# Attention in units of 64 tokens of all four batches, in place of 256 tokens of one, in a fused attention and two-MLP kernel

## The reference

```python
f = 1.0 / (1.0 + np.exp(-f_logit))
for t in range(S):                      # gated linear attention
    state = f[:, :, t, :, None] * state + np.einsum('bhd,bhe->bhde', k[:, :, t], v[:, :, t])
    y[:, :, t] = np.einsum('bhd,bhde->bhe', q[:, :, t], state)
x = y.transpose(0, 2, 1, 3).reshape(3072, 384)
x = ((1/(1+np.exp(-(x @ w_gate)))) * (x @ w_val)) @ w_out      # 384 -> 1536 -> 384
h = x @ w_in                                                   # 384 -> 2048
out = (h * (1/(1+np.exp(-1.702 * h)))) @ w_out2                # 2048 -> 384
```

## Time and profile before

| | us |
|---|---|
| three runs, median | 945.4 (943.34 to 945.67) |
| the profiled execution | 943.24 |
| its span | 941.5 |
| TensorE busy in the span | 928.0 (99%), 7197 matmuls |
| VectorE, ScalarE, GpSimd busy | 453.3, 375.1, 114.3 |
| first matmul of the first MLP | at 27.71 |

### The profile page before, as it was taken

One profiled execution on the slowest core, in us unless ns is written; L12 is line 12 of the kernel. 1 busy time (PEld: TensorE's weight loads), 2 busy tenths in 40 slices (PEclk: granted clock), 3 DMA queues, 4 the chain that ended last, 5 costly groups with the idle time before them and its releaser, 6 DMA issues.

```text
span 941.5 us, 18155 instructions
## 1 busy us (share of the span) xinstructions
PE 928.0 (99%) x7197; PEld 776.5 (82%) x7197; DVE 453.3 (48%) x886; ACT 375.1 (40%) x917; POOL 114.3 (12%) x125
## 2 busy tenths in 40 slices
PE   7999999999999999999999999999999999999997
PEld 5899988888888888888888888888888888888886
DVE  7787775456546544753333243343443443343433
ACT  4765654444444434443334342333232233332332
POOL 4222221101112110210014420000000000000000
PEclk8999999999999999999999999999999999999999
DMA  5852322112211221120123320020100200200000
GB/s 144 244 158 71 89 68 74 43 47 82 56 46 41 76 59 44 56 55 12 59 84 102 101 67 1 1 68 1 45 23 1 68 1 1 67 1 1 35 1 36
DMA packets 44008, 52.36 MB, mean 56 GB/s; under 512 B 8464, under 2 KB 33808, under 8 KB 43920
## 3 DMA queue, kind: packets, MB, share of 16 engines
q1 hardware_dynamic: 41488, 43.53, 16.2%
q10 hardware_dynamic: 2432, 7.62, 2.7%
HBM read 36.96 MB, written 9.44 MB: 49 GB/s over the span
## 4 chain that ended last, share of the span: by engine, by line
PE 94%; DVE 2%; SPq 1%; DMA 1%; issue 1%; ACT 0%; DVEq 0%; ACTq 0%
PE up_ps L1094 17%; PE up_ps L1096 17%; PE up_ps L1095 17%; PE out_ps L1094 13%; PE out_ps L1095 12%; PE out_ps L1096 12%; PE att_ps L1042 2%; PE att_ps L1064 1%; PE att_ps L1054 1%; PE att_ps L1087 1%; PE turn_ps L1021 1%; DMA x_raw<-y_t 1%; PE out_ps L1006 1%; SPq L411 0%; PE att_ps L1076 0%
## 5 line engine op out<-in xcount | busy, mean ns | idle before, releaser
L1094 PE MATMUL up_ps<-x_hi,w_hi 128*128 128x512 f32 (+1 forms) x792 | 293.3, 370 | 0.1
L1096 PE MATMUL up_ps<-x_hi,w_lo 128*128 128x512 f32 (+1 forms) x792 | 293.0, 370 | 0.0
L1095 PE MATMUL up_ps<-x_lo,w_hi 128*128 128x512 f32 (+1 forms) x792 | 292.9, 370 | 0.0
L1094 PE MATMUL out_ps<-act_hi,w_hi 128*128 128x512 f32 (+1 forms) x540 | 207.7, 385 | 0.7 <-DVE act_lo L938 0.7
L1095 PE MATMUL out_ps<-act_lo,w_hi 128*128 128x512 f32 (+1 forms) x540 | 202.8, 376 | 0.0
L1096 PE MATMUL out_ps<-act_hi,w_lo 128*128 128x512 f32 (+1 forms) x540 | 202.4, 375 | 0.0
L715 ACT CAST act_hi<-act_f 128x512 fp32r<-128x512 f32 (+1 forms) x180 | 106.6, 592 | 233.5 <-DVE act_f L924 161.1
L1094 PEld LDWEIGHTS up_ps<-x_hi,w_hi 128*128 128x128 f32 x792 | 149.2, 188 | 25.5 <-ACT act_f L709 0.3
L1096 PEld LDWEIGHTS up_ps<-x_hi,w_lo 128*128 128x128 f32 x792 | 149.2, 188 | 25.4
L1095 PEld LDWEIGHTS up_ps<-x_lo,w_hi 128*128 128x128 f32 x792 | 149.2, 188 | 25.1
L938 DVE TENSOR_TENSOR act_lo<-act_f,act_hi 128x512 fp32r<-128x512 f32 (+1 forms) x180 | 117.6, 653 | 79.4 <-ACT act_hi L715 79.4
(11 more groups left out here) (84 smaller groups left out, 573.6 us busy)
## 6 DMA issues: line engine op xcount, KB each, us to landing
stage<-w SPq DMA_DIRECT2D x16, 384.0 KB, 3.3
stage<-w ACTq DMA_DIRECT2D x9, 576.0 KB, 4.3
k_raw<-k_t SPq DMA_DIRECT2D x96, 48.0 KB, 1.9
q_raw<-q_t SPq DMA_DIRECT2D x96, 48.0 KB, 1.9
v_raw<-v_n SPq DMA_DIRECT2D x48, 96.0 KB, 2.4
x_raw<-x_dram SPq DMA_DIRECT2D x6, 768.0 KB, 4.7
out_t<-final SPq DMA_DIRECT2D x18, 256.0 KB, 2.3
f_raw<-f_t SPq DMA_DIRECT2D x88, 48.0 KB, 2.0
```

What stands on the lines that cost most here:

```text
L1094: pe.matmul(dst, w_hi[:, at:at + P], m_hi, start=first, stop=False)
L1095: pe.matmul(dst, w_hi[:, at:at + P], m_lo, start=False, stop=False)
L1096: return pe.matmul(dst, w_lo[:, at:at + P], m_hi, start=False, stop=last)
```

## The change

A unit is now one pair and 64 tokens of each of the four batches (CH = B = 4, W still 256). Its four chunks are of different batches and don't depend on each other; each continues from the state that the same pair had one step, that is four units, earlier. There are still 48 units in 12 steps. What follows in the code:

- The states of a pair stand in place (`state[:, pair, :, :]`). VectorE decays all four by one instruction as soon as the unit's gate products are there (`decay_state`), and adds the products of k and v by one more (`new_state`). TensorE reads the decayed state, with q_dec itself: `q_in`, `prepare_q`, `no_state` and the 4 chained instructions are gone.
- A visit is a pair (turned, made); the products for the states and the outputs are of one unit. There are 8 visits before the first block, one kind each (turned alone, made alone), 5 in the first group (j = 0, 2, 4, 6, 8), and then 8 a group. Every `made` beyond the first 4 units uses the L1087 way, with the state's part in columns of its own; the first 4 units have no state and no such matmuls. TensorE runs one warm matmul after each of the 8 visits and 12 before the first block.
- The gates of the first 4 units are written to PSUM (`up_ps`) and scanned from there. So TensorE waits for the scans before the first block. GpSimd sets `q_raw` and `gate` to 0, not VectorE.
- f, k and q are loaded with 4 runs of 64 tokens a row, v by two DMAs, not one, x2 is stored by one DMA a slab and step of 64 tokens of four batches (6 for a group of 512 where it were 3). The second MLP's group 0 needs five groups stored, and all later ones need all seven.
- The first four loads of v go to ScalarE's queue; the first piece of w1 goes from ScalarE's to SyncE's; SyncE's order before the first block is new.

```diff
-    W = 256
     C = 64
     SIDES = P // C
-    BLOCKS = W // P
-    CH = W // C
-    STEPS = TOK // W
+    CH = B
+    W = CH * C
+    BLOCKS = CH // SIDES
+    STEPS = S // C
...
-    VISITS = [(0, None, None), (1, 0, None), (2, 1, 0), (3, 2, 1), (None, 3, None), (None, None, 2), (None, None, 3),
-              (4, None, None), (5, 4, None)]
-    VISITS += [(n, n - 1, n - 2) for n in range(6, UNITS)] + [(None, UNITS - 1, UNITS - 2), (None, None, UNITS - 1)]
-    BEFORE_MLP = 7
+    VISITS = []
+    for n in range(UG):
+        VISITS += [(n, None), (None, n)]
+    BEFORE_MLP = len(VISITS)
+    VISITS += [(UG, None)] + [(n, n - 1) for n in range(UG + 1, UNITS)] + [(None, UNITS - 1)]
...
-        for j in (0, 1, 2, 4, 6, 8) if g == 0 else (0, 1, 3, 4, 5, 7, 8, 9):
+        for j in (0, 2, 4, 6, 8) if g == 0 else (0, 1, 3, 4, 5, 7, 8, 9):
...
+        def gate_of(n):
+            return up_ps[:, n % 2, 0:SPACED] if n < UG else gate[:, n % 2, :]
...
+        def stores_before(group):
+            return 16 * (GROUPS1[group][0] // W if group < NG1 else STEPS + group - NG1)
...
-                            sp.dma_start(f_raw[rows[i], u.s, :], f_t[u.pair, i, :, u.tokens]).then_inc(f_loaded[u.s], 16)
+                            sp.dma_start(by_batch(f_raw[rows[i], u.s, :]), f_steps[u.p, i, :, :, u.tokens]).then_inc(f_loaded[u.s], 16)
...
-                        sp.dma_start(v_raw[:, n % 4, :, :],
-                                     v_n[u.pair, :, u.third * BLOCKS:(u.third + 1) * BLOCKS, :]).then_inc(v_loaded[n % 4], 16)
+                        for r in range(SIDES):
+                            sp.dma_start(v_raw[halves[r], n % 4, :, :], v_chunks(u, r)).then_inc(v_loaded[n % 4], 16)
...
+                            for m, step in enumerate(steps_of(group)):
+                                sp.dma_start(x2_steps[:, k, :, step, :], by_batch(final[:, k, m * W:(m + 1) * W])).then_inc(stored[k], 16)
...
 # ScalarE, before the first block
                 first_load_f(2)
+                first_load_v(0)
                 forget(1)
-                take_end(0)
                 first_load_f(3)
+                first_load_v(1)
                 take_k(0)
                 forget(2)
+                first_load_v(2)
+                take_end(0)
+                forget(3)
+                first_load_v(3)
...
+                take_y(2)
+                first_move_y(2, slice(0, 2))
+                take_end(3)
+                w1_first_part(0)
                 take_y(3)
-                first_move_y(3, slice(None))
-                w1_first_part(0)
+                first_move_y(3, slice(0, 1))
...
+                def decay_state(n):
+                    u = Unit(n)
+                    if u.step:
+                        dve.wait_ge(state_done, n - UG + 1)
+                        dve.wait_ge(after_done, n + 1)
+                        dve.tensor_tensor(state[:, u.p, :, :], state[:, u.p, :, :],
+                                          chunks(after_prod, u.s)[:, :, 1].unsqueeze(2).to_broadcast([P, CH, D]),
+                                          ALU.mult).then_inc(state_decayed, 1)
...
-                    for c in range(CH):
-                        products = banks(v)[:, c % SIDES, KV_COL + c // SIDES * D:KV_COL + (c // SIDES + 1) * D]
...
+                    products = banks(v)[:, :, KV_COL:KV_COL + BLOCKS * D].rearrange("p r (c d) -> p r c d", c=BLOCKS)
+                    if u.step:
+                        dve.wait_ge(state_decayed, n - UG + 1)
+                        dve.tensor_tensor(by_side(state[:, u.p, :, :]), by_side(state[:, u.p, :, :]), products,
+                                          ALU.add).then_inc(state_done, 1)
+                    else:
+                        dve.tensor_copy(by_side(state[:, u.p, :, :]), products).then_inc(state_done, 1)
...
 # TensorE, in a visit
-                    if made is not None and v < APART:
-
-                        last.then_inc(tiles_done, 1)
-                        pe.wait_ge(tiles_done, made + 1)
...
+                    if made is not None and m.step:
+
+                        pe.wait_ge(state_decayed, made - UG + 1)
...
 # TensorE, before the first block
-                    keep_warm({0: 2, 1: 3, 4: 2}.get(v, 0))
+                    keep_warm(1)
 
                 wait_y(pe, 3)
-                keep_warm(4)
-                for slot in (1, 2):
+                keep_warm(3)
+                for slot in (0, 1, 2):
                     pe.wait_ge(y_moved[slot], 16 * moves(slot, UG))
-                    keep_warm(4)
-                pe.wait_ge(x_hi_done, 1)
-                keep_warm(2)
+                    keep_warm(3)
+
+                pe.wait_ge(scan_done, UG)
+                pe.wait_ge(state_done, UG)
```

More of the change, by code:

```diff
@@ L447, in _ @@
                 load_f(6)
[L448 removed]
                 load_v(5)
+                load_kq(6)
                 load_f(7)
@@ L604, in first_load_f, with first_load_v @@
                     for i in range(PAIR):
-                        act.dma_start(f_raw[rows[i], u.s, :], f_t[u.pair, i, :, u.tokens]).then_inc(f_loaded[u.s], 16)
+                        act.dma_start(by_batch(f_raw[rows[i], u.s, :]), f_steps[u.p, i, :, :, u.tokens]).then_inc(f_loaded[u.s], 16)
+                def first_load_v(n):
+                    u = Unit(n)
+                    for r in range(SIDES):
+                        act.dma_start(v_raw[halves[r], n % 4, :, :], v_chunks(u, r)).then_inc(v_loaded[n % 4], 16)
                 def take_k(n):
@@ L717, in _ @@
                     if b.first_mlp and (b.g, b.j) in VISIT_AT:
-                        turned, _, made = VISITS[VISIT_AT[b.g, b.j]]
+                        turned, made = VISITS[VISIT_AT[b.g, b.j]]
                     if turned is not None:
                         take_k(turned)
-                    if made is not None and copied_first(out_visit[made]):
-                        take_y(made)
-                    if turned is not None:
-                        prepare_q(turned)
                     if b.first_mlp and (b.g, b.j) in FORGET_AT:
@@ L728, in _ @@
                         take_end(PREPARE_AT[b.g, b.j])
-                    if made is not None and not copied_first(out_visit[made]):
+                    if made is not None:
                         take_y(made)
@@ L943, in _ @@
                         end_decay(ahead)
+                        decay_state(ahead)
                     if b.q < J1 and b.j + 2 < J1:
                         w1_second_part(b.j + 2)
-                    if v is not None and v >= APART and VISITS[v][2] is not None:
-                        add_y(VISITS[v][2], v)
+                    if v is not None and VISITS[v][1] is not None:
+                        add_y(VISITS[v][1], v)
                     if b.first_mlp and b.g < NG1 - 1 and b.j == SPLIT_AT1:
@@ L1053, in visit @@
                                 for i in range(PAIR):
-                                    last = pe.matmul(ps[halves[i], r, at], k_rows[halves[r], kept % 2, c, halves[i]],
-                                                     v_raw[halves[r], kept % 4, c, cols[i]], start=opens and c == 0,
+                                    last = pe.matmul(ps[halves[i], r, at], k_rows[halves[r], made % 2, c, halves[i]],
+                                                     v_raw[halves[r], made % 4, c, cols[i]], start=False,
                                                      stop=False, skip_group_check=True)
-                        opens = False
                     if turned is not None:
```

268 lines of the change are left out of this document (111 added, 157 removed).

## The result

| | before | after |
|---|---|---|
| median of 6 runs, us | 943.95 (943.34 to 945.67) | 955.35 (954.13 to 958.31) |
| profiled execution, us | 943.24 | 954.32 |
| its span, us | 941.5 | 952.2 |

The changed kernel takes 1.012 of the time before (95% interval 1.0102 to 1.0137): 1.2% slower, where 0.7% faster was forecast. It lies outside the range of 930.5 to 944.5.

A forecast was written before the change was run, and what follows sets the result against it. TensorE, busy 99% of the span, was taken as the bound, with gains only at the start and first group. From 943.24, -5.2 - 3.5 + 2.0 gave 936.5, stated as 937.5 since runs lie 0 to 2.2 above; range 930.5 to 944.5.

The forecast's parts named there:

- part 3: Second group: the second v load delays SyncE's queue, its last y move and TensorE; 2.0 us lost, ends 0 and 4.
- part 1, before the first block: Start of the kernel: first block begins at 22.5, not 27.71, with ends 20.5 and 26; 5.2 us won.
- part 2, the first group: First group of blocks: waits and the two-pass order go, visits take 1.37 us; 3.5 us won, ends 2 and 4.3.
- At nothing: Fewer ScalarE instructions, shorter VectorE work behind 85 us, short-run x2 stores and later load_x2 in group 1: no change in time.
- the forecast's own price of an issue: SyncE's queue, second group: the second v load adds 0.42 + 0.05 us in each of 8 visits, 3.8 us.
- y 3 at 18.2: ScalarE before the first block: the copy of y 3 comes at 18.2, after the last state at 16.8.
- Rival B: Start hardly shorter: ScalarE's queue or half-clock warm matmuls set the first block at 26; about 941 to 944; chance 0.13.
- Next late is VectorE's low part of w1, 0.4 to 0.5: First group, third block: VectorE's low part of w1 comes late, losing 0.4 to 0.5 us, once.
- Gates in PSUM: Start: scans 0.71 and GpSimd products 0.68 throughout; if not so, 0.4 lost on each of three scans, 1.2 us.
- C: Slower rival: a DMA packet costs 59 ns at any size, delaying the start and second group; 949 to 951; chance 0.08.
- the fitted line: DMA packet cost, all loads: 4 ns + 0.052 ns a byte, so 18 ns for a 256 B run.
- D: Rival: new waits in every visit for the decayed state, 40 visits of 0.2 us, +8; about 946; chance 0.04.

The follow-up runs named there:

- a_v1: The changed kernel with v laid out by unit in DRAM, one DMA of 128 rows of 768 B for two of 64 rows; 942.45 us, ratio 0.9984.
- a_vact: The changed kernel with the second group's v loads issued from ScalarE's queue, not SyncE's, same 64 rows; 944.76 us, ratio 0.9996.
- b_v2c: The kernel before with each v load cut by columns into two DMAs of 128 rows of 384 B; 951.03 us, ratio 1.0062.
- b_v2: The kernel before with each v load cut into two DMAs of 64 rows; 955.35 us, ratio 1.0109.
- c_order: `a_v1` with unit 4's sigmoid behind the y copies, y moves and first w1 piece, its scan behind the last state; 940.76 us, ratio 0.9963.
- d_w1: `c_ofp` with the second w1 piece's load issued behind the moves of y 2; 939.06 us, ratio 0.9931.
- d_dve: `c_ofp` with VectorE making low parts of w1's first piece and x before unit 4's scans, ScalarE's take_end(4) behind x; 937.35 us, ratio 0.992.
- c_gsb: `a_v1` with the first four units' gates back in SBUF, their 0 columns set by VectorE; 941.65 us, ratio 0.9975.
- a_fkq: The changed kernel with f, k and q rows as one run of 1 KB, not four of 256 B, same number of DMAs; 952.89 us, ratio 1.0083.
- c_ofp: `c_order` with unit 5's sigmoid behind the third w1 piece, and f, k and q each one DMA of 128 rows of 1 KB; 938.89 us, ratio 0.994.

## Why the prediction was wrong

Part by part, in us (part 3 is from the second visit of the second group to 150.42):

| | forecast | ends | measured |
|---|---|---|---|
| part 1, before the first block | -5.2 | -7.2 to -1.7 | +0.86 |
| part 2, the first group | -3.5 | -4.3 to -2 | -0.53 |
| part 3, SyncE's queue, second group | +2.0 | 0 to 4 | +9.27 |
| at nothing | 0 | | +0.69 |
| sum | -6.7 | | +10.28 |

Part 3 turned the change into a loss, and most of this section is on it. Parts 1 and 2, the whole of the forecast gain, failed as well: without part 3's loss, as in `a_v1` and `a_vact`, the kernel is about as fast as before, and not 0.7% faster.

**Part 3, the failed step.** "I take 2.0 lost, ends 0 and 4": SyncE's queue in the second group. The mechanism was named right, link by link. The size was wrong: pauses of 0.88 and 5.75 are nearly all of the 6.60, and 2.67 more of half clock follow, 9.3 together. Three errors are in it. By `b_v2c`, the forecast's own price of an issue costs 3.1 to the start of the next group, not 2.0; that less of the queue's waits could be used than was counted is the likely reason, and not shown. The same run has 1.6 of half clock, which the forecast had not priced at all, though the earlier trace rows shows 0.50 behind a stretch of pauses. And the 64-row issue takes 0.66, not 0.42: within the kernel before, the 0.60 of `b_v2` costs 2.9 more than the 0.43 of `b_v2c`, and in the kernel after, by difference, some 4.6 of the 9.3 are left for it and for the slower issues of k and q, if the two kernels' queues compare. The forecast took 0.42 for it from issues of 128 and of 48 rows; that no row of before had 64 rows was the reason to give it a bound above, and it got none. The argument that a 128-row piece issues faster than a 48-row load was true and still said nothing about 64 rows. That the step decides the loss is shown from both sides: `a_vact` and `a_v1` take the loss out of the changed kernel, `b_v2` puts it in the kernel before.

**Part 1, -5.2 forecast, +0.86 measured.** The fourth k was decayed at 14.09 without a wait for its DMA, near the 13 forecast. What failed came behind: "y 3 at 18.2", measured 23.02. Timeline of ScalarE, after:

```profile
5.23 1.45 ACTq L619 DMA_DIRECT2D v_raw<-v_n  x2
...
12.78 0.95 ACTq L614 DMA_DIRECT2D f_raw<-f_t  x2
...
19.39 0.42 ACT L602 ACTIVATE gate<-f_raw 128x256 f32<-128x256 f32 x1 [3.53 <-DMA f_raw<-f_t]
...
23.02 0.36 ACT L638 COPY y_t<-out_ps 128x256 f32<-128x256 f32 x1
...
32.59 0.42 ACT L602 ACTIVATE gate<-f_raw 128x256 f32<-128x256 f32 x1 [5.30 <-DMA f_raw<-f_t]
```

A pair of v loads takes 1.24 to 1.45, not 0.81. Then the sigmoid of unit 4 waits 3.53 for an f that lands 6.11 behind its issue, while two w1 pieces of 576 KB, issued at 10.84 and 12.36, are under way; the copies of k 3 and of the last two y stand behind it in ScalarE's order. The forecast had no term for that wait. The 12 warm matmuls before the first block took 5.1 (23.43 to 28.57), near the 4.7 of the half clock. One more thing had no term: the clock was low far earlier than the forecast took it, from 8 us and not from 16. Windows of the kernel after:

```profile
6.00:8.00 2.00, 1.29 (x20) 0.82 (x20) 0.93 (x4) 0.39 (x1) 0.68 (x2) 1.00 0.75 160
...
10.00:12.00 2.00, 2.00 (x36) 1.58 (x32) 0.91 (x3) 0.49 (x2) 0.10 (x1) 0.50 0.65 148
```

What it cost on its own no run shows. Here it mostly hid behind the wait for f: in `a_v1`, whose clock is whole until 18 us, that wait is there too and the last y is copied at 22.23, only 0.8 earlier. `c_order`, `d_w1` and `d_dve` show that the start had a row of such limits close behind each other: with v, f, k and q in half the DMAs and the sigmoids and VectorE's list moved, it begins at 22.18 (`d_dve`), near the forecast, and with the w1 piece moved too at 21.05. Rival B named ScalarE's queue and the half clock and put the first block at 26, with a chance of 0.13; it came at 28.57, and the time lies outside B's as well.

**Part 2, -3.5 forecast, -0.53 measured.** The visits are as short as forecast: two blocks with one visit take 7.94 in the rows (41.45 to 49.39), against 7.9. They even save more than forecast, as the first group has five visits and not six, and the sixth, 0.7, is only put off (see below). The stretch from the first block to 84 us still gave back 0.53 only. The last row of ScalarE's timeline above is why: the sigmoid of unit 5 waits 5.30 for its f, w1's third high part and the block's own sigmoid stand behind it, TensorE pauses 2.86 at 34.47, and the next 5 us run at 0.66 of the clock in the mean, which by the 45 matmuls from 34.47 to 41.45 (6.98 us, where 5.5 are usual at 0.12 each) is another 1.5. "Next late is VectorE's low part of w1, 0.4 to 0.5" was so the wrong successor in the kernel after; in `a_v1`, where that pause is 0.21, the wait for the low part is there, with 1.47, where 0.4 to 0.5 were forecast.

**Gates in PSUM.** Right in both durations, 0.71 and 0.68 side by side, against up to 1.16 and 0.93 with both inputs in SBUF. The loss that it avoids was put at 1.2 and isn't to be seen in the time of `c_gsb`. With that, the rule of the Trainium skill (GPSIMD Engine Reference, Specifications) that VectorE and GpSimd contend when a VectorE instruction has two inputs in SBUF agrees with a trace for both sides.

**At nothing.** No wait of TensorE above 0.7 us lies behind 150 us, and the distance to the kernel before stays at 9.60 up to 449.64, so these held. One small thing was missed. The kernel after runs its units later against the blocks, so its last visits are fuller: it still transposes at 455.90, where the visit of before at 446.38 has none, and +0.69 is lost between 449.64 and 464.43. That is the visit that the first group no longer holds.

**Rivals.** C needed 45 ns a packet. The page of after gives 952.2 x 16 x 0.182 / 103312 = 26.8 ns for 423 B on average, where the fitted line says 26; a k load lands in 2.1 us, not 1.9. The direction of C was right and its cause was not. The Trainium skill (DMA: Bandwidth & Descriptors, Specifications) says that transfers below 512 B miss the full rate because of a read-modify-write. The transfers of q1, most of them loads from DRAM, don't show such a price: their 26.8 ns lie on the line, which has none, and all that `a_fkq` leaves to the short runs is about 2.5 us in 955. For D, the decayed state, TensorE never waits.

What stays open: that a DMA of 64 rows issues in 0.66 us and one of 128 rows in 0.43 was measured, not explained. And the cause of the hole of 2.41 us in `c_ofp` isn't shown. It was gone in `d_w1`, when a 576 KB load was issued later, but in `d_dve`, which issues that load as early as `c_ofp`, the last y came 1.6 earlier too; each was seen in one profile.

## What to carry to other kernels

Before an edit adds an issue to a queue that has no gaps on the path, take its duration from a DMA of the same rows and shape, or give it an end well above the others: a quarter of a microsecond more for each of two issues is 4 us over eight visits. A long pause of TensorE can cost more than its length (5.75 cost 2.7 more, 3.17 cost 1.6 more), so price the slow clock behind it too. An earlier first block is worth only what the next blocks don't give back: 5.4 us earlier came out as 2.5. And a load that is small lands late when large ones are under way, so what needs it must not stand ahead of the path's own work in an engine's order.

## What the runs showed of the hardware

- Time to issue a DMA on SyncE's queue, medians from 84 to 128 us: 0.42 for 48 rows of k or q of one run each, 0.44 for four runs each (0.42 again in `a_fkq`); 0.42 to 0.44 for 128 rows of v, in 384 B or 768 B; 0.60 for 64 rows of v of one run (`b_v2`), 0.66 for two runs (after); 0.59 for a move of y. On ScalarE's queue 0.63 for 64 rows of v. Bytes did not order them. Shape isn't all either: the pair of f loads behind a move of y has the shape of k and took 0.58 and 0.44 (at 129.30 in the kernel after).
- Pauses of 5.75, 5.58, 3.17 and 2.86 us of TensorE between blocks were each followed by 0.50 of the clock for about 3 to 6 us, with 2.7, 2.1, 1.6 and 1.5 us lost; behind pauses of 2.51 (`a_vact`, at 37.42), 2.20 (`a_fkq`, at 33.26), 1.86 (`a_v1`) and 0.88 the clock stayed at 1.00.
- A 48 KB load landed in 6.1 and 6.5 us beside two w1 pieces of 576 KB, against 2.1 as a rule.
- A scan of VectorE with one input in PSUM and a product of GpSimd ran side by side at 0.71 and 0.68; with both scan inputs in SBUF (`c_gsb`), the one that began second took 1.16 (scan) or 0.93 (product).
